# A column-attention and gated feed-forward kernel: seven late blocks, four of them in three split passes; tile 0's token sums by accumulating DMAs; the first M in two banks; the softmax by halves

## What is computed

```python
def _attn_ref(q, k, v, tau):                     # q, k, v: (2, 6016, 256), fp32
    qn = q / (np.linalg.norm(q, axis=1, keepdims=True) + 1e-06)
    kn = k / (np.linalg.norm(k, axis=1, keepdims=True) + 1e-06)
    s = kn.transpose(0, 2, 1) @ qn / tau         # (2, 256, 256)
    s = s - s.max(-1, keepdims=True)
    a = np.exp(s)
    a /= a.sum(-1, keepdims=True) + 1e-09
    return (v @ a).astype(np.float32)

def _moe_ref(x, w_in, w_out, alpha):             # x: (12032, 256), d_ff = 2048
    h = x @ w_in
    g = np.maximum(h, 0.0) + alpha * np.minimum(h, 0.0)
    return (g @ w_out).astype(np.float32)
```

## Time and profile before

| | |
|---|---|
| median of 3 runs | 1076.53 us (1076.34 to 1077.75) |
| the profiled execution's own time | 1076.63 us |
| its span, first to last instruction | 1074.8 us |
| TensorE busy | 1070.9 us |
| VectorE busy | 847.0 us |
| ScalarE busy | 654.6 us |
| TensorE's granted clock, mean | 1.00 of full speed |

### The profile page before, as it was taken

The page is one execution under the profiler, slowest core; times in us unless marked ns, Lnnn a source line. Parts: engine busy times, 40 slices in busy tenths (PEclk is TensorE's granted clock), DMA queues, the critical chain, the costliest instruction groups (busy, mean ns, idle before and its releaser), DMA issues.

```text
span 1074.8 us, 13902 instructions
## 1 busy us (share of the span) xinstructions
PE 1070.9 (100%) x4995; PEld 906.2 (84%) x4995; DVE 847.0 (79%) x1349; ACT 654.6 (61%) x1100; POOL 40.4 (4%) x54
## 2 busy tenths in 40 slices
PE   9999999999999999999999999999999999999998
PEld 7888888888888888888998888888888888888898
DVE  6999987877877777787798887777777777787776
ACT  6676677667766555655666655555555555555544
POOL 0000000000000000000000000000000000000000
PEclk9999999999999999999999999999999999999999
DMA  9621154455453102103212101201202202200101
GB/s 382 284 88 50 40 158 127 138 160 150 134 162 99 30 13 54 45 9 79 69 30 73 50 11 49 59 8 52 59 1 59 59 0 54 57 1 10 40 1 35
DMA packets 30837, 80.07 MB, mean 74 GB/s; under 512 B 2992, under 2 KB 9264, under 8 KB 29232
## 3 DMA queue, kind: packets, MB, share of 16 engines
q1 hardware_dynamic: 24288, 67.80, 18.1%
q0 software_dynamic: 6336, 11.28, 6.8%
q10 hardware_dynamic: 144, 0.11, 0.0%
HBM read 64.04 MB, written 12.32 MB: 71 GB/s over the span
## 4 chain that ended last, share of the span: by engine, by line
PE 100%; ACT 0%; issue 0%; POOL 0%; POOLq 0%
PE y_ps L538 47%; PE x_ps L512 24%; PE z_ps L512 12%; PE p_ps L512 6%; PE x_ps L444 4%; PE s_ps L464 3%; PE p_ps L498 2%; PE s_ps L444 1%; PE y_ps L498 1%; PE y_ps L553 0%; PE z_ps L440 0%; PE p_ps L486 0%; PE p_ps L473 0%; PE p_ps L479 0%; ACT y_stage L876 0%; PE s_ps L435 0%
## 5 line engine op out<-in xcount | busy, mean ns | idle before, releaser
L538 PE MATMUL y_ps<-g_hi,w_hi 128*128 128x512 f32 (+1 forms) x760 | 293.1, 386 | 0.0
L538 PE MATMUL y_ps<-g_hi,w_lo 128*128 128x512 f32 (+1 forms) x760 | 292.9, 385 | 0.0
L538 PE MATMUL y_ps<-g_lo,w_hi 128*128 128x512 f32 (+1 forms) x760 | 292.9, 385 | 0.0
L757 ACT CAST g_hi<-h 128x512 fp32r<-128x512 f32 (+1 forms) x384 | 234.0, 610 | 78.6 <-DVE h L1011 69.3
L1011 DVE SCALAR_TENSOR_TENSOR h<-h,small_sb 128x512 f32<-128x512 f32 (+1 forms) x384 | 273.7, 733 | 0.0
L1003 DVE SCALAR_TENSOR_TENSOR h<-z_ps,sigma_neg,h 128x512 f32<-128x512 f32 (+1 forms) x192 | 141.7, 738 | 148.0 <-ACT h L747 147.6
L1045 DVE TENSOR_TENSOR g_lo<-h,g_hi 128x512 fp32r<-128x512 f32 (+1 forms) x384 | 249.9, 670 | 0.8 <-ACT g_hi L757 0.5
L747 ACT ACTIVATE h<-x_ps,sigma_neg 128x512 f32<-128x512 f32 (+1 forms) x192 | 130.7, 681 | 175.2 <-PE x_ps L512 165.1
L747 ACT ACTIVATE h<-x_ps,sigma 128x512 f32<-128x512 f32 (+1 forms) x192 | 130.6, 680 | 124.8 <-PE x_ps L512 120.2
L538 PEld LDWEIGHTS y_ps<-g_hi,w_hi 128*128 128x128 f32 x760 | 142.7, 188 | 27.3 <-issue 0.3
L538 PEld LDWEIGHTS y_ps<-g_hi,w_lo 128*128 128x128 f32 x760 | 142.7, 188 | 27.0
(11 more groups left out here) (129 smaller groups left out, 1009.4 us busy)
## 6 DMA issues: line engine op xcount, KB each, us to landing
rows_t<-qk_t SPq DMA_DIRECT2D x32, 376.0 KB, 4.0
stage<-qk SPq DMA_DIRECT2D x10, 1024.0 KB, 13.3
v_stage<-v_t SPq DMA_DIRECT2D x20, 512.0 KB, 4.6
y_t<-y_stage SPq DMA_DIRECT2D x20, 512.0 KB, 2.8
pair<-qk SPq DMA_DIRECT2D x19, 512.0 KB, 3.7
v_stage<-v_t POOLq DMA_DIRECT2D x27, 256.0 KB, 4.1
scratch<-w_in SPq DMA_DIRECT2D x12, 256.0 KB, 2.8
v_stage<-v_stage POOLq DMA_DIRECT2D x9, 256.0 KB, 3.3
```

The source lines that it names most:

```text
L538: product = nc.tensor.matmul(y_ps[t][oc][:, 0:H], w_part[:, j, ws], g_part[:, k, 0:H], start=jp == 0 and k < 2 and w_part is w_hi and g_pa ...
L757: nc.scalar.copy(g_hi[:, k, 0:H], h[:, k, 0:H]).then_inc(g_hi_ready, 1)
```

## The change

- `LATE` goes from 9 to 7, so batch 1 has 20 pairs instead of 19. The first four late blocks are split into high and low parts (`split_late_hi`, `split_late_lo`) and multiplied in three passes, the other three stay unsplit. The low part is written over `late` itself.
- Batch 0's pieces are 1, 2, 3, ten of 4, 1 instead of 2, 3, ten of 4, 2.
- Tile 0's T1 to T4 come from GpSimd's accumulating DMAs, like those of the other tiles; `mix_first_v` is gone. B21 now stands before T2 in every tile's order.
- A first M now lies in the same half of two banks, its lower and its upper rows apart, and `make_m` reports each half (`m_half_done`); `take_m` of the first M copies the first half while the second is made.
- The row maximum is taken for each half of the scores, and each exponential waits for its half alone.
- In group 0 the third M comes before the z product, the last late block alone stays in the group; T2 and T4 of tile 0 are waited for only where they are used. Between the second M and group 0 no late block is left.
- Smaller moves: the w_out splits (`W_AT`), the load of tile 1's tokens behind the first w_in slices, the table loads of the softmax of batch 1, the M mix of group 1, and the g_lo split at the start of group 1.

```diff
-    B11, B22, T1, T3, T2, B21, T4 = range(7)
+    B11, B22, T1, T3, B21, T2, T4 = range(7)
...
-    PIECES = [2, 3] + [4] * 10 + [2]
+    PIECES = [1, 2, 3] + [4] * 10 + [1]
...
-    LATE = 9
-    LATE_PARTS = (4, 5)
+    LATE = 7
+    LATE_PARTS = (4, 3)
+
+    LATE_SPLIT = 4
...
-        m_ps = (*y_ps[0], *y_ps[1])
+        m_ps = [[y_ps[jp % 2][kc][:, jp // 2 * C:(jp // 2 + 1) * C] for kc in range(CC)] for jp in range(M_FIRST)]
...
-        W_AT = {1: (6, 7), 2: (8, 9), 3: (10, 11), 4: (12, 13), 6: (14, 15)}
+        W_AT = {1: (5, 6), 2: (7, 8), 3: (9, 10, 11), 4: (12, 13), 6: (14, 15)}
...
-            for T in range(1, ALL):
+            for T in range(ALL):
...
+            def split_late_block(n):
+                pe.wait_ge(late_lo_ready, n + 1)
+                for kc in range(CC):
+                    ks = slice(C + kc * P, C + (kc + 1) * P)
+                    for k_part, q_part in ((late_hi, late_hi), (late_hi, late_lo), (late_lo, late_hi)):
+                        nc.tensor.matmul(S[:, kc * C:(kc + 1) * C], k_part[:, n, ks], q_part[:, n, 0:C],
+                                         start=False, stop=False, skip_group_check=True)
...
-                product.then_inc(m_done, 1)
+                    product.then_inc(m_half_done, 1)
...
-            late_blocks(0, 4)
+            for n in range(LATE_SPLIT):
+                split_late_block(n)
+            late_blocks(LATE_SPLIT, LATE - 2)
             transpose_probs(0)
-            late_blocks(4, 5)
+            late_blocks(LATE - 2, LATE - 1)
             for jp in range(2):
                 make_first_m(jp)
-            late_blocks(5, LATE - 2)
...
             def exponentials(b):
-                act.wait_ge(max_ready, b + 1)
                 for kc in range(CC):
+                    act.wait_ge(max_ready, CC * b + kc + 1)
...
+            def split_late_lo(n):
+
+                dve.wait_ge(late_hi_ready, n + 1)
+                nc.vector.tensor_tensor(late_lo[:, n, :], late[:, n, :], late_hi[:, n, :].bitcast(fp32),
+                                        ALU.subtract).then_inc(late_lo_ready, 1)
...
-                step(nc.vector.reduce_max(row_max, scores, AX_X))
-                nc.vector.tensor_scalar(neg_max, row_max, -1.0, None, ALU.mult).then_inc(max_ready, 1)
+                for kc in range(CC):
+                    step(nc.vector.reduce_max(row_max[:, kc:kc + 1], scores[:, kc, :], AX_X))
+                    nc.vector.tensor_scalar(neg_max[:, kc:kc + 1], row_max[:, kc:kc + 1], -1.0, None, ALU.mult
+                                            ).then_inc(max_ready, 1)
...
+                if G == 1:
+                    split_g_lo(G - 1, 3)
                 add_part(G, Y, 0).then_inc(c11_done, 1)
-                if G > 0:
+                if G > 1:
                     split_g_lo(G - 1, 3)
```

More of the change, by code:

```diff
@@ L679, in split_pair_hi, with split_late_hi @@
                 nc.scalar.copy(pair_hi[:, :, :], pair[:, :, :]).then_inc(pair_hi_ready, 1)
+            def split_late_hi(n):
+                act.wait_ge(late_loaded[0], 16)
+                nc.scalar.copy(late_hi[:, n, :], late[:, n, :]).then_inc(late_hi_ready, 1)
             def take_root(b):
@@ L715, in take_m @@
                 n = JP * b + jp
-                mf, bank = (mf0, mf1)[jp % 2], m_ps[jp] if b == 0 and jp < M_FIRST else Y
-                act.wait_ge(m_done, n + 1)
+                mf, halves = (mf0, mf1)[jp % 2], m_ps[jp] if b == 0 and jp < M_FIRST else y_halves
+                if n > 0:
+                    act.wait_ge(m_half_done, CC * (n + 1))
                 if n >= 2:
```

128 lines of the change are left out of this document (61 added, 67 removed).

## The result

The changed kernel took 1078.91 us (median of 16 runs, 1077.89 to 1079.75), the kernel before 1077.07 us in as many (1076.34 to 1078.03). The ratio is 1.0017 with a 95% interval of 1.0011 to 1.0023: slower by 1.8 us. That is just under the 0.2% within which the prediction called a time the same, though the interval reaches over it. The prediction was 1075.8 with a range up to 1077.4. So the sign was wrong and the time lies outside the range. The profiled execution took 1078.46 us, with a span of 1076.6 us, 1.8 over the one before.

A forecast was written before the change was run, and what follows sets the result against it. TensorE, busy 1070.9 of 1074.8 us, was taken to bound the kernel. The terms -0.8 - 0.1 + 0.35 + 0.35 + 0.1 + 0.3 - 0.9 summed to -0.7 us, giving 1075.8, range 1074.5 to 1077.4.

The forecast's parts named there:

- Term 2: At the start: a first piece of one block lands earlier and closes TensorE's 0.2 us hole; -0.1 us (0 to -0.2).
- Term 1: TensorE's work: six blocks change from unsplit to three passes, 0.86 to 0.73 us each; -0.8 us.
- Term 3: First M: VectorE reaches at_lo about 0.45 us later, so TensorE's hole grows from 0.32 to about 0.67; +0.35 us (0 to +0.7).
- Term 4: Second M to first up matmul: no unsplit blocks cover the chain to m_lo any more; +0.35 us (0 to +0.8).
- Term 5: Tile 0's sums by DMA: T1 fits ahead of the exponentials, T2 and T4 stand in ScalarE's queue; +0.1 us (0 to +0.8).
- Rival B: T1's DMA lands late, holding ScalarE, exponentials, transposes and first M; chance 0.03 of 2.15 us or more, 0.08 over 1 us.
- Term 6: Groups 1 to 4: a third w_lo in group 3 and TensorE's earlier arrival in group 2; +0.3 us (0 to +1.0).
- Term 7: Three mended orders against x-copy waits (0.6), plus the z_ps (0.2) and transpose (0.1) waits; -0.9 us (0 to -1.2).
- rival C: Tile 0 eats the head's lead as VectorE waits in groups 2 to 5, over 1 us; 1076.5 to 1077.5, chance 0.2.
- rival A: At at_lo and M the thin covers hold, terms 3 to 6 near 0; 1074.7 us, chance 0.2.

The follow-up runs named there:

- e3: The changed kernel with the old pieces (2, 3, ten of 4, 2) put back: 1077.87 us, ratio 1.0011 to the kernel before.
- f1: The kernel before with only the new pieces (1, 2, 3, ten of 4, 1): 1078.23 us, ratio 1.0015.
- j1: The kernel before with pieces 1, 2 and eleven of 4: 1077.87 us, ratio 1.0012.
- c3: The kernel before with only the new table-load order and the g_lo split ahead of the first sum in group 1: 1076.39 us, ratio 0.9998.
- e1: The changed kernel with the M mix of group 1 back ahead of the slope: 1078.73 us, ratio 1.0017 to the kernel before.
- h2: The kernel before with pieces 2, 2, 3 and ten of 4: 1077.13 us, ratio 1.0001.
- j4: The changed kernel with the old pieces, T1's DMA issued earlier and the M mix of group 1 as before: 1077.12 us, ratio 1.0008 to the kernel before.
- j3: e3 with B11's low part made earlier, so that T1's DMA is issued earlier: 1077.52 us, ratio 1.0008 to the kernel before.

## Why the prediction was wrong

**Term 2 (the first block, -0.1) is the step that failed most plainly, but not alone:** without the new pieces e3 is still 1.3 us over the kernel before beside it, and terms 6 and 7 below miss 1.15 us together. Term 2 priced the new pieces by TensorE's first hole alone, and put at nothing what they do to the pieces behind them. The runs show +1.5 for the pieces by themselves (f1) and 0.6 to 1.0 of the changed kernel's loss (e3). The cost takes two ways, both from a third piece that lands late, in the seven profiles with 1, 2, 3 between 7.76 and 9.13 where the rate of the kernel before (five blocks at 6.47, 0.62 us for one more) gives an estimated 7.1: TensorE's fourth block waits for it, and with it the rq broadcast and all behind (j1, and most of what parts e3 from the changed kernel), and VectorE's additions of squares begin late and move the clamp (f1). For the clamp the prediction counted a block more alone, "the clamp of 41.92 moves to about 42.7"; it came at 43.01, released by TensorE's channel sums.

**Term 1 (TensorE's work, -0.8) and the saving ahead of group 1 held.** Group 0 starts 0.2 us and group 1 1.0 us before the time of the kernel before, in spite of an rq broadcast 0.2 us later; 20 pairs and 7 late blocks are all there.

**Term 3 (at_lo, +0.35) was right in kind,** the matmuls on at_lo at 53.70, released by it, after a wait of 0.5 of their weight load; at_lo itself stands at 52.96, later than the 52.68 forecast, by the late clamp. **Term 4 (M, +0.35) was nearly right as a wait,** TensorE idled 0.43 us for m_lo. But the first up came at 56.78, 0.6 later than forecast, by what the start and at_lo had brought in: the second multiplication began at 54.95, where 55.05 was to be its end, and m_lo at 56.07, where 56.15 was to be its end.

**Term 5 (T1's DMA, +0.1) is right for the profiled execution of the changed kernel and wrong in its margin.** "So it fits, by about 0.3 us at the median" took the landings of tiles over which the page shows the DMA engines at most half busy. Rival B, priced at 0.08 for over a microsecond, was there in its mild form in seven of the eight variants with these sums (ScalarE held 0.5 to 1.5 us; TensorE's transposes came up to 0.9 us later from the rq broadcast than in the changed kernel). Its strong form was in none. How often it holds the changed kernel's unprofiled runs can't be read; its median lies 0.45 over its profiled execution.

**Term 6 (groups 2 to 4, +0.3) was low by 0.7 us.** Group 2 lost 0.7 at the x copy and group 4 0.35 at its M (105.71 for a start that fitted 105.35). **Term 7 (-0.9) gave about a half:** the table loads 0.26, the z wait 0.2; the g_lo order alone only moved a wait from the x to the z product (c3), and with the moved M mix it gave 0.26 in group 1, while the mix moved the next wait into group 2, so e1 came out even. The new waits of groups 2 to 4 add to the 1 us that the prediction gave as the sign of rival C, though the first of them is released by ScalarE. Its reading, that VectorE in tile 0 takes back what the change frees on TensorE, fits them.

**The sum.** The hi by hi matmuls into p_ps, one in each group, with first and last start, are now

```profile
L532 PE MATMUL p_ps<-v_hi,m_hi x96: 362/389/467, 56.8 to 1059.4; 128*128 128x512 f32 x80, 128*128 128x448 f32 x16
```

and the same instructions of the kernel before run from 57.0 to 1057.8: 1002.6 us for 1000.8. The pair more (+1.46), the block and the z wait that left group 0 (-0.8), the g_lo order and the moved mix in group 1 (-0.26) and the table loads (-0.26) make +0.1. The new waits in groups 2 and 4 make 1.05. The rest, some 0.6, sits in the last tile, of matmuls of 448 columns: from group 88 to group 95 it took 65.12 us in this execution and 64.57 before. That comes and goes between executions (65.11 in h2, which has the old orders, 64.80 in e3, which has the new ones), so I take it for no part of the change. With pieces, T1 and mix mended (j4), 0.7 us are left over the kernel before (0.9 by the ratio), in an interval that includes none. So the 0.8 us of work went into waits in the head and in tile 0, and the pieces came on top. Of the 0.6 to 1.0 us that they cost in the medians, the changed kernel's own profile shows only the 0.2 by which its rq broadcast is late; how the loss of 1.8 divides is known to a few tenths at best.

Three numbers of the prediction are slips that decide nothing: in the earlier trace rows the longest landing is 1.1 us over the median and not 1.2, by rival B's own date of 48.5 a landing of 8 us costs 3.2 and not 3.3, and rival A stands at 1074.7 in one place and 1074.5 in another.

## What to carry to other kernels

When pieces are cut anew, read when each of the next pieces lands, not only when the first matmul starts: a piece that lands late holds TensorE at once, and a saturated helper chain that begins with the first loads (the additions of f1) carries it to a date 30 us later. Take a DMA's landing from rows with the same load on the DMA engines; here T1's landed in 4.1 us at the median and in up to 6.8 us beside w_out's load. And where VectorE has 0.3 us to spare, work taken off TensorE can come back as waits; an order that mends one hole has to be followed to the next.

## What the runs showed of the hardware

A DMA of two blocks (512 KB) issued behind one of a single block (256 KB) was followed by slower packets in each of eight profiles, 299 to 403 GB/s from 4 to 8 us, and no other order of the same bytes was (426 to 435 in ten profiles). And DMAs that add, issued from GpSimd while the DMA engines were full, landed 4.5 to 7.9 us after their issue, and 4.0 to 4.2 at the median of all tiles; issuing T1's 1.2 us earlier brought its landing forward by 0.55 (e3 to j3).

TensorE's first matmuls of 256 columns take 0.43 us a step in most profiles and later ones 0.22, and the number of slow ones differs with no relation to when they began: from 4.38 and 4.40 on, 30 matmuls took 7.91 us in the changed kernel, with five steps of 0.43, and 35 took 7.96 in e3, with none:

```profile
4.40 7.96 PE L453 MATMUL x_ps<-stage 128*128 128x256 f32 x35 [0.17 <-DMA stage<-qk]
```

The trace's clock record tells these two apart. It begins with 1.00, the level of 2.4 GHz, at 6.65 us in the changed kernel and at 3.73 in e3, ahead of its first block. In all 18 profiles it begins between 3.7 and 6.9 us, and no step of 0.43 starts behind it. What was granted ahead of it no record says; a step twice as long would fit the level of 1.2 GHz. TensorE had been issuing since 1.00 us in both.

So up to a microsecond between two profiles can be this alone. Comparing them from the rq broadcast on takes it out, but takes out too what the pieces cost on TensorE.
